# Bucketed attention and two MLPs: regrouping TensorE's work in each attention step, moving the head splits and a projection, and loading two columns by DMA

## The reference

```python
q_bits = (einsum('bhsd,dk->bhsk', q, proj) > 0)      # 6 bits, k likewise
mask   = bucket(q_bits)[..., :, None] == bucket(k_bits)[..., None, :]
scores = where(mask, q @ k.T / sqrt(D), -1e9)
attn   = exp(scores - max);  attn /= sum(attn) + 1e-9
x      = (attn @ v) as [1536, 512]
h = x @ w_in;  g = P(h) / (Q(h) + 1e-6);  x = g @ w_out   # P cubic, Q quadratic
h = x @ w_in2; g = h * clip(h + 3, 0, 6) / 6;  out = g @ w_out2
```

## Time and profile before

| | |
|---|---|
| median of 3 runs | 782.55 us (782.19 to 782.91) |
| the profiled execution, its own time | 782.55 us |
| its span, first to last instruction | 780.8 us |
| PE / PEld busy | 759.1 us (97%) / 583.4 us (75%) |
| DVE / ACT / POOL busy | 486.0 (62%) / 439.5 (56%) / 215.3 us (28%) |
| attention: first scores at, MLPs' first matmul at | 13.31 us, 245.03 us |

### The profile page before, as it was taken

One profiled execution on the slowest core, in us unless ns is written; L12 is line 12 of the kernel. 1 busy time (PEld: TensorE's weight loads), 2 busy tenths in 40 slices (PEclk: granted clock), 3 DMA queues, 4 the chain that ended last, 5 costly groups with the idle time before them and its releaser, 6 DMA issues.

```text
span 780.8 us, 11273 instructions
## 1 busy us (share of the span) xinstructions
PE 759.1 (97%) x3712; PEld 583.4 (75%) x3712; DVE 486.0 (62%) x794; ACT 439.5 (56%) x783; POOL 215.3 (28%) x366
## 2 busy tenths in 40 slices
PE   4799999999999999999999999999999999999998
PEld 2666666666666788888888888888888888888886
DVE  4777777777765788889888988861222312232223
ACT  2676677777766788877666888861221212222121
POOL 1655566666663254300000154450000000000000
PEclk9999999999999999999999999999999999999999
DMA  6544455443320123200000133320000100010001
GB/s 148 143 114 106 92 133 129 98 125 93 77 60 1 55 87 102 82 0 0 0 0 0 28 92 97 108 81 0 1 1 0 54 0 0 0 55 0 1 1 54
DMA packets 35084, 43.31 MB, mean 55 GB/s; under 512 B 4192, under 2 KB 23392, under 8 KB 35040
## 3 DMA queue, kind: packets, MB, share of 16 engines
q1 hardware_dynamic: 34752, 42.32, 20.5%
q10 hardware_dynamic: 288, 0.43, 0.2%
HBM read 26.61 MB, written 3.15 MB: 38 GB/s over the span
## 4 chain that ended last, share of the span: by engine, by line
PE 89%; issue 2%; DVE 2%; ACT 2%; DMA 1%; POOL 1%; SPq 1%; ACTq 0%; POOLq 0%; DVEq 0%
PE y_ps L920 33%; PE h_ps L866 11%; PE h_ps L867 11%; PE h_ps L868 11%; PE o_ps L846 8%; PE t_ps L829 7%; PE s_ps L819 4%; PE s_ps L820 3%; ACT probs L448 2%; DVE neg_max L618 1%; DMA probs<-in_k 1%; PE p_ps L803 1%; DVE q_cross L613 1%; PE p_ps L846 1%; POOL exp_bias L397 0%
## 5 line engine op out<-in xcount | busy, mean ns | idle before, releaser
L866 PE MATMUL h_ps<-x_hi,slot 128*128 (+1 forms) x384 | 149.8, 390 | 0.0
L867 PE MATMUL h_ps<-x_lo,slot 128*128 (+1 forms) x384 | 149.5, 389 | 0.0
L712 DVE SCALAR_TENSOR_TENSOR t_abs<-t_abs,h_ps 128x512 f32<-128x512 f32 x48 | 33.0, 689 | 187.1 <-ACT t_abs L520 187.1
L868 PE MATMUL h_ps<-x_hi,slot 128*128 (+1 forms) x384 | 149.5, 389 | 0.0
L520 ACT ACTIVATE t_abs<-h_ps,three_col 128x512 f32<-128x512 f32 x48 | 33.1, 689 | 191.5 <-PE h_ps L868 191.5
L410 POOL TENSOR_TENSOR slot<-w_raw,slot 128x512 fp32r<-128x512 f32 x64 | 81.6, 1293 | 207.0 <-ACT slot L475 206.9
L920 PE MATMUL y_ps<-g_hi,slot 128*128 128x512 f32 x384 | 126.2, 390 | 0.0
L920 PE MATMUL y_ps<-slot,g_hi 128*128 128x512 f32 x384 | 118.2, 389 | 0.0
L448 ACT ACTIVATE probs<-s_ps,exp_bias,exp_scale 128x768 f32<-128x768 f32 x96 | 95.0, 990 | 32.9 <-POOL exp_bias L397 31.5
L618 DVE TENSOR_REDUCE neg_max<-s_ps 128x1 f32<-128x768 f32 x96 | 91.6, 954 | 18.1 <-PE s_ps L820 15.0
L829 PEld LDWEIGHTS t_ps<-ident,probs 128*128 128x128 f32 x576 | 63.5, 143 | 46.4 <-issue 26.2
(11 more groups left out here) (71 smaller groups left out, 1138.4 us busy)
## 6 DMA issues: line engine op xcount, KB each, us to landing
w_raw<-in_moe_w_in SPq DMA_DIRECT2D x32, 256.0 KB, 2.7
w_raw<-in_moe_w_out SPq DMA_DIRECT2D x32, 256.0 KB, 2.8
raw<-in_q SPq DMA_DIRECT2D x16, 192.0 KB, 3.2
v_nat<-in_v SPq DMA_DIRECT2D x16, 192.0 KB, 3.2
raw<-in_k SPq DMA_DIRECT2D x15, 192.0 KB, 3.5
k_main<-q_main SPq DMA_DIRECT2D x15, 192.0 KB, 2.6
k_cross<-q_main SPq DMA_DIRECT2D x15, 192.0 KB, 3.2
k_cross<-q_cross SPq DMA_DIRECT2D x15, 192.0 KB, 2.6
```

Of the source, the lines that this page charges most:

```text
L866: mm(h_ps[b][:, :], w_hi, x_hi[:, kt, cols], start=(kt == 0), stop=False)
L867: mm(h_ps[b][:, :], w_hi, x_lo[:, kt, cols], start=False, stop=False)
L868: last = mm(h_ps[b][:, :], w_lo, x_hi[:, kt, cols], start=False, stop=(kt == KT - 1))
```

## The change

It has four parts.

1. **PE's step.** The transposes come straight behind the scores; `weigh` and `project` come after them. `weigh` runs in three groups of two contraction tiles for each half, at t = 1, 3, 5, in place of five groups (one, one, two, one, one) at t = 1 to 5. In the last pair three groups of two take the place of four groups. `project` moves from j = 0 to j = 1, and so `threshold` from j = 1 to j = 2.
2. **ACT.** `split_hi` moves from t = 2 (behind `take_turned`) to t = 0 (ahead of `take_turned`).
3. **DVE.** `split_lo` moves from t = 3 to t = 1.
4. **The start.** POOL makes two rows of 128 values in one partition with four fills. ACT waits for them and issues two DMAs, each of which spreads a row over the 128 partitions of a column of `bit_col`. DVE's reduction is gone and its wait is for the DMAs.

```diff
-    WEIGH_AT = {1: (0,), 2: (1,), 3: (2, 3), 4: (4,), 5: (5,)}
-    PROJECT_AT = 0
+    WEIGH_AT = {1: (0, 1), 3: (2, 3), 5: (4, 5)}
+    PROJECT_AT = 1
-    LAST_WEIGH = {1: (0, (0,)), 2: (0, (1, 2)), 3: (0, (3,)), 4: (0, (4, 5)),
-                  6: (1, (0,)), 7: (1, (1, 2)), 8: (1, (3,)), 9: (1, (4, 5))}
+    LAST_WEIGH = {1: (0, (0, 1)), 2: (0, (2, 3)), 4: (0, (4, 5)), 6: (1, (0, 1)), 8: (1, (2, 3)), 9: (1, (4, 5))}
...
-            nc.gpsimd.memset(bit_sel[:, 0, :], TINY).then_inc(sel_made, 1)
-            nc.gpsimd.memset(bit_sel[:, 1, :], 1.0).then_inc(sel_made, 1)
+            nc.gpsimd.memset(bit_row[:, 0, :], TINY).then_inc(sel_made, 1)
+            nc.gpsimd.memset(bit_row[:, 1, :], 1.0).then_inc(sel_made, 1)
             pool.wait_ge(sel_made, 2)
-            below(0, BITS, 0.0)
-            below(1, MASKROWS, -PENALTY)
-            pool.wait_ge(sel_made, 4)
-            below(0, 3 * BITS, TINY)
-            below(1, QUAD, 1.0)
+            least, value = (bit_row[:, c, :].rearrange("o (c r) -> o c r", r=QUAD) for c in range(2))
+            nc.gpsimd.memset(least[:, :, BITS:3 * BITS], 0.0).then_inc(sel_made, 1)
+            nc.gpsimd.memset(value[:, :, MASKROWS:QUAD], -PENALTY).then_inc(sel_made, 1)
...
             act.dma_start(swapped[0:D, :], k_dram[dram_head(0, 0), :, :]).then_inc(swapped_in, 16)
+            act.wait_ge(sel_made, 4)
+            for c in range(2):
+                act.dma_start(bit_col[:, c:c + 1], bit_row[0:1, c, :]).then_inc(bit_col_in, 16)
             nc.scalar.preload_act_table_set("natural_log_exp_and_others")
...
                 if n >= 1:
                     exponentials(n - 1, j - 1)
+                if t == 0 and h + 2 < NHEAD:
+                    split_hi(h + 2)
                 if n >= TURN_LAG:
                     take_turned(n - TURN_LAG)
-                if t == 2 and h + 2 < NHEAD:
-                    split_hi(h + 2)
...
-                if t == 3 and h + 2 < NHEAD:
+                if t == 1 and h + 2 < NHEAD:
                     split_lo(h + 2)
...
-            dve.wait_ge(sel_made, 6)
-            nc.vector.tensor_reduce(bit_col[:, :], bit_sel[:, :, :], AX.X, ALU.min).then_inc(bit_col_made, 1)
...
-            dve.wait_ge(bit_col_made, 1)
+            dve.wait_ge(bit_col_in, 32)
             threshold(0, slice(0, D), first=True)
...
                 scores(h, i, u, n, j, t)
+                if n >= TURN_LAG:
+                    for half in range(2):
+                        turn_probs(n - TURN_LAG, half)
                 if i == PAIRS - 1 and j in LAST_WEIGH:
                     weigh(i - 1, *LAST_WEIGH[j])
...
-                if n >= TURN_LAG:
-                    for half in range(2):
-                        turn_probs(n - TURN_LAG, half)
```

More of the change, by code:

```diff
@@ L105, in bucket_attention_and_two_mlps @@
         proj_pair = sb("proj_pair", [P, QUAD])
-        bit_sel = sb("bit_sel", [P, 2, P // QUAD])
+        bit_row = sb("bit_row", [1, 2, P])
         bit_col = sb("bit_col", [P, 2])
@@ L164, in bucket_attention_and_two_mlps @@
         poly_in = sem("poly_in")
-        bit_col_made = sem("bit_col_made")
+        bit_col_in = sem("bit_col_in")
         swapped_in = sem("swapped_in")
@@ L364, in alone @@
                 pool.sem_inc(pool_waits, 1)
[L367 to L371, removed]
-            nc.gpsimd.memset(bit_sel[:, 0, :], TINY).then_inc(sel_made, 1)
-            nc.gpsimd.memset(bit_sel[:, 1, :], 1.0).then_inc(sel_made, 1)
-            pool.wait_ge(sel_made, 2)
-            below(0, BITS, 0.0)
-            below(1, MASKROWS, -PENALTY)
-            pool.wait_ge(sel_made, 4)
-            below(0, 3 * BITS, TINY)
-            below(1, QUAD, 1.0)
+            nc.gpsimd.memset(bit_row[:, 0, :], TINY).then_inc(sel_made, 1)
+            nc.gpsimd.memset(bit_row[:, 1, :], 1.0).then_inc(sel_made, 1)
+            pool.wait_ge(sel_made, 2)
+            least, value = (bit_row[:, c, :].rearrange("o (c r) -> o c r", r=QUAD) for c in range(2))
+            nc.gpsimd.memset(least[:, :, BITS:3 * BITS], 0.0).then_inc(sel_made, 1)
+            nc.gpsimd.memset(value[:, :, MASKROWS:QUAD], -PENALTY).then_inc(sel_made, 1)
             nc.gpsimd.memset(ident[:, :], 0.0).then_inc(sel_made, 1)
@@ L383, in _ @@
             nc.gpsimd.memset(three_col[:, :], 3.0).then_inc(sel_made, 1)
-            pool.wait_ge(sel_made, 9)
+            pool.wait_ge(sel_made, 5)
             nc.gpsimd.affine_select(out=ident[:, :], in_=ident[:, :], compare_op=ALU.not_equal, fill=1.0,
@@ L881, in step @@
                     project(i + 1, 1)
-                if n >= TURN_LAG:
-                    for half in range(2):
-                        turn_probs(n - TURN_LAG, half)
             project(0, 0)
             project(0, 1)
-            pe.wait_ge(sel_made, 10)
+            pe.wait_ge(sel_made, 8)
             for i in range(PAIRS):
```

## The result

| | before | after |
|---|---|---|
| median | 782.73 us (782.19 to 782.98, 4 runs) | 788.10 us (786.96 to 789.28, 4 runs) |
| the profiled execution, its span | 782.55, 780.8 us | 787.28, 785.5 us |
| ratio of the times | | 1.0069, 95% interval 1.0054 to 1.0084 |

The account below looks back on a forecast made before the run. PE, 97% busy, bounds the kernel, but uneven steps expose waits. Pair 2 +0.25, pairs 3 to 6 +3.6, pair 1 -0.45, last pair -0.8, start +0.5: +3.1 on 782.55, 785.65 us; range 776.5 to 789.5.

Parts of the forecast that it names:

- groups: PE's weigh: 26 groups fewer at 0.25 us each, 1.00 us off a full pair, 6.5 us in all.
- t = 0 and 1: First two steps of a head: ACT's upper_x and split_hi make them 5.07 us instead of 4.37.
- DVE's copy: Short steps: the copy ends about when PE wants its bank; 0.15 us lost a head.
- early half: POOL's slot one step after j = 7: scores wait 1.0 us in each of pairs 3 to 6.
- pair 1: The pair with head 2, which has no upper_x and so no loss at its first steps: -0.45 us.
- last pair: Final attention pair: -0.50 us for groups and -0.3 for smaller waits, -0.8 together.
- columns land, first scores: Start: the columns sent by DMA land at 9.2 us, first scores move to 15.1.
- start in all, to pair 1: Later first scores lose 1.8 us, moved project and threshold regain 1.3: +0.5 us together.
- The shared port: DVE's split_lo at t = 1 meets POOL's normalise: 3 us more for 13 heads, left out of the sum.
- PE's count alone: Rival: queues absorb the uneven steps, waits stay, only the groups are gone: -6.6 us, 776 us; chance 0.20.
- The early halves: Rival: ACT's and DVE's terms hold, POOL's 1.0 us is mostly absorbed: -0.9 us, 781.7 us; chance 0.18.
- late columns: Rival at the start: columns land at 12 us rather than 9.2, +2.8 us more, 788.5 us; chance 0.12.

Follow-up runs that it names:

- e8: e7 with the old tables of five groups, four in the last pair: 782.78 us, ratio 1.0003.
- e7: Changed kernel, old start, split_hi behind take_turned, DVE's copy first, exponential ahead of upper_x, first early half at j = 8: 776.1 us.
- e1: Kernel before with only the changed kernel's two tables of groups: 784.0 us, ratio 1.0014.
- e3: Changed kernel with ACT's split_hi at t = 0 behind take_turned: 786.69 us, ratio 1.0049.
- e5: Changed kernel with DVE's take_turned right behind the maximum, ahead of the inverse and lower_x: 785.34 us, ratio 1.0034.
- e6: Changed kernel with the edits of e3 and e5 together: 781.16 us, ratio 0.9981.
- e2: Changed kernel with the two threshold columns made as before, by POOL's selects and DVE's reduction: 784.63 us, ratio 1.0027.
- e10: Kernel before with the new start alone, columns carried by two DMAs: 785.34 us, ratio 1.004.
- e4: Changed kernel with the first early half at j = 8 in place of 7: 784.69 us, ratio 1.0027.
- e9: e7 with split_lo at t = 1 held until exp_bias of the same tile is made: 777.87 us, ratio 0.9943.

## Why the prediction was right, and where its sizes were off

Direction and mechanism came as forecast: uneven steps whose cover falls short. The size did not: +3.1 was forecast and +5.4 measured, and within the sum some terms are right only because errors cancel. The forecast in its own terms against the profile after:

| term | predicted | measured |
|---|---|---|
| groups | -1.00 a pair, -6.5 | -0.95 a pair, -6.7 (e8 against e7) |
| `project` beside `weigh` | -0.10 | about -0.10 (4.20 - 3.42 = 0.78; before, 2.30 - 1.42 = 0.88) |
| t = 0 and 1, without `project` | 5.07 | 5.05 (1.63 + 3.42) |
| DVE's copy | 0.15 a head | 0.16 in each of three further long steps, 0.48 a pair; at t = 1 beside ACT's |
| `threshold` | +0.20 a pair | 0.08 at j = 4 (1.47; j = 10, without it, 1.40); not tested by a run |
| pair 2 | 28.9 | 29.03 |
| early half | +1.0 | +0.74 |
| pairs 3 to 6 | 29.9 | 29.76 |
| pair 1 | -0.45 | +0.14 |
| last pair | -0.8 | -0.10 |
| columns land, first scores | 9.2, 15.1 | 9.73, 15.70 |
| start in all, to pair 1 | +0.5 | +0.94 |
| last scores to MLPs | not in the sum | +0.25 |

**Groups.** Right in size, as far as e8 and e7 can be compared, but this is not a gain that stands by itself. e1 has it without the moved splits and is slower than before.

**t = 0 and 1.** The length was right and the cause half of it. The prediction named ACT's order, and valued DVE's copy at 0.15 beside it. In truth either copy alone holds the step, at 3.42 or 3.36, so mending one gives 0.06 or nothing there (e3, e5), and both 0.4 a head (e6). The sum hid this: two delays in parallel were added as if they were in series. That it came out for pair 2 is luck: DVE's copy, taken once a head, bites in three long steps more.

**DVE's copy in long steps.** The working, copy done at S + 2.55 against a bank wanted at 2.53, holds for every short step, not only for t = 0. Those three waits are 0.48 a pair; the prediction counted 0.30, at t = 0 and 1. With the copy ahead of the inverse 0.26 of them goes (e5); the maximum still stands ahead of it.

**Early half.** The wait at j = 11 is 0.88 (2.27 against 1.39), all but the predicted 1.0; then 0.13 come back, as in a step that starts late DVE's copy is done in time (3.01 after it, 3.14 elsewhere). A delay that is followed by a smaller one swallows it; the prediction didn't look one step on.

**Pair 1 and the last pair** failed, by 0.6 and 0.7. "Head 2 has no `upper_x` and so none of it": it has 1.45 and 4.20 at t = 0 and 1, of which only the first is shorter (1.64 in pair 2), since `split_hi` still stands ahead of ACT's copy. That is 0.5 above the 4.37 that the prediction took as free. "Waits that are smaller" in the last pair: `lower_x` is there at t = 0, j = 5 and j = 10, ahead of the copy, and in its first two steps

```profile
221.54 0.54 DVE L634 TENSOR_TENSOR x_lo<-o_ps,x_hi 128x384 fp32r<-128x384 f32 x1
...
221.99 0.55 DVE L628 COPY pt_second<-t_ps 128x384 f32<-128x384 f32 x1
...
222.69 0.52 PE L821 MATMUL t_ps<-ident,probs 128*128 128x128 f32 x3 [0.16 <-DVE pt_second L628]
```

the transposes wait for DVE with no split anywhere: 3.36 where 2.98 is free. With DVE's copy first that step takes 3.02 and the pair 25.95 (e5), 0.86 under the kernel before, which is the forecast's -0.8.

**The start.** The wait is the one named, and from bits to scores it is 5.97 (predicted 5.95). The columns were 0.5 later than taken. The prediction put them near the transfer ahead of them, at 8.3; with the change that transfer is there by 7.01, and they still came at 9.73. The sum of +0.5, measured +0.94, is luck. It was made of +1.8 lost and 1.3 regained. With the new orders and the old start (e2), pair 1 begins 3.27 us sooner than in the kernel before (38.45 against 41.72), and the new start puts it 4.21 later (42.66). Both terms were more than twice what was taken, and part of both is the matmuls' length in pair 0 (last section). Taken alone the start costs 3.5 us by e2 and 2.7 by e10.

**The shared port.** It was weighed and left out. In this kernel that was right, though not as the prediction pictured it: `split_lo` starts first (119.99 to 120.94 in pair 3) and is not delayed, and `normalise` beside it takes 1.62 (120.11 to 121.73), yet the next `exp_scale` waits for a maximum until 122.66. Where other waits are gone, the split meets `exp_bias` instead, and that costs 0.47 a pair (e6) and 0.65 (e7).

**The rivals.** PE's count alone would have given 776; e7 reaches that time only after five mendings. The early halves did bite, and e4 takes their 0.74 a pair back. The median is near the late columns' 788.5, but not for their reason: they came at 9.73, not at 12, and short of the 10.3 from which their rival decides.

The median is 2.45 us above the 785.65 of the forecast. Of this, 1.6 comes from these terms (span +4.7 against +3.1), most of it pair 1, the last pair, the start and the stretch to the MLPs, with pairs 3 to 6 shorter than forecast; 0.8 is there because the profiled execution was quicker than the median of its kernel (787.28 against 788.10).

## What to carry to other kernels

Making steps uneven saved time here only once every engine's queue carried the short step. Write for each engine what stands ahead of the instruction that frees a buffer, and put that instruction first. When two engines free two halves of one resource, mend both before judging either. A long VectorE operation on two SBUF inputs needs a place in which GpSimd has nothing urgent, and late work that can wait (here the normalisation) is the right one to delay.

## What was not expected of the hardware

- VectorE's split and GpSimd's work on SBUF don't run side by side: the one that starts second ends behind the first, and a short instruction loses most by it, measured by its own length. A bias of 0.26 us took 0.90 and ended 0.13 behind the split (e7). A normalisation of 0.91 took 1.62 and ended 0.79 behind the split (after). A split of 0.94 took 1.65 and ended 0.80 behind the normalisation (e9).
- Two column DMAs of 128 pieces, issued from 2.91 us on, took 5.8 to 6.1 us to land among the first loads.
- In every trace the scores' first matmul takes 0.76 us or more in the first step and 0.47 to 0.50 later. In the kernel before it changes between 24.0 and 28.8 us (below), after the change by 25.1, in e2 by 17.8, and the granted clock is 1.00 from 14 to 28 us in the kernel before. In e10 the same matmul takes 0.80 at 26.33, where the granted clock is 0.50. So early matmuls have the length of the lower level under a row that shows 1.00; whether they ran at it isn't shown. What sets the moment stays open, and it moves pair 0 by a microsecond or more between kernels. From the kernel before:

```profile
24.01 0.80 PE L819 MATMUL s_ps<-k_cross,q_cross 128*128 128x512 f32 x1
...
26.59 0.64 PE L819 MATMUL s_ps<-k_cross,q_cross 128*128 128x512 f32 x1
...
28.81 0.47 PE L819 MATMUL s_ps<-k_cross,q_cross 128*128 128x512 f32 x1 [0.43 <-ACT probs L448]
```
